# An early weight cast, a narrower wait and two earlier low parts in a Strassen-form attention and feed-forward kernel

## The chip, the cores and the metric

The kernel runs on one core of one Trainium2 chip. The metric is the device time of one execution in microseconds (us); lower is better. A number of executions are timed and the median is told; one more is recorded by the hardware profiler, and all rows shown here are of that one.

## What is computed

Attention with a soft cap, then two feed-forward layers, all in float32. The second and third steps take nearly all of the matrix work:

```python
scores = cap * np.tanh(scores / cap)            # 4 batches, 12 heads, 448 x 448
attn = exp(scores - max) / (sum + 1e-09)
x = (attn @ v)                                  # as 1792 tokens x 768
h = np.maximum(np.maximum(x @ w1, x @ w2), x @ w3)
x2 = h @ w_out                                  # 768 -> 768
g, val = x2 @ w_gate, x2 @ w_val                # 768 -> 1536
out = (g * sigmoid(g) * val) @ w_out2           # 1536 -> 768
```

## The kernel before

After the attention part, which the change does not touch, the work is 60 **quads**, two times 30 (one half of the tokens each). A quad is a 2 x 2 block product done with seven products in place of eight (Strassen in Winograd's form); product i of quad q is called (q, i) here, i from 0 to 6. Each product has three chunks of depth 128, and each chunk three matmuls of 448 columns, because a float32 operand is split into a high and a low part: `hi*hi`, `hi*lo`, `lo*hi`. So a product is 9 matmuls and a quad 63.

What a product needs:
- **A weight.** SyncE loads it into `whole` (a ring of 10), ScalarE casts the high part (`weights_hi`, L588), GpSimd subtracts to get the low part (L461). The load of weight n is issued once product n - 10 is done. ScalarE casts weight n + 8 at product n of its own list.
- **Operands.** A stage's input is seven blocks per chunk, in the order B11, T1, T2, T3, B22, B21, T4 (`SPLIT_ORDER`). T1 to T4 are differences that VectorE makes (L742 to L753). Each is split as well: ScalarE makes the high part (`operand_hi`, L606), VectorE the low part (`operand_lo`, L760: two inputs in SBUF).
- **A free PSUM bank.** Products 0 to 3 go to banks 0 to 3; products 4, 5 and 6 are added onto banks 0, 2 and 3, after ScalarE has copied bank 0 out (`take_p1`, L612), VectorE has made `u4` (L858) and VectorE has made the block C22 (L864). Ahead of these VectorE makes `u2` (L851) from product 1 and ScalarE's copy. So within a quad VectorE's chain is u2, u4, C22, later C12 (L880) and C21 (L887); `u2` and `u4` gate (q, 5), and C22 gates (q, 6).

Nothing reorders the work at run time: each engine runs the list that the code writes out, and semaphores join them. A quad whose result feeds the next stage is called a chunk's last quad; its event e is (stage, chunk). The seven low parts of event e are spread by hand over VectorE's list: some right after T4 is made, two after the next quad's `u2`, two after its `u4`, and what is left after its C22.

A **stage start** is a quad with q mod 30 in 0, 9, 12, 18, 27. The stage's last chunk of operands is not ready then, so TensorE runs the first two chunks of (q, 0) to (q, 3), then of (q+1, 0) and (q+1, 1), and then the third chunks. It so needs weight (q+1, 1) early.

Kinds of quads in one half: 0 to 8 "max" (three projections, their maximum), 9 to 11 "out1", 12 to 17 "gate" and "val" in turn, 18 to 20 "part", 21 to 26 gate and val again, 27 to 29 "out". In a gate quad ScalarE's list has the tanh of C22 (L644) ahead of the weight cast of product 5. In an out1 quad ScalarE copies C11 straight into the operand block B11 (`take_c11`, L628).

Of the kernel before, what the change touches and what calls it, by code (L numbers as in the profile page):

```python
# [28 lines left out]
PROD = 7  # L29
BANK_OF = (0, 1, 2, 3, 0, 2, 3)  # L30
J_B11, J_T2, J_T1, J_T3, J_B21, J_B22, J_T4 = range(PROD)
# [72 lines left out]
def event_of(q):  # L104

    s, k = divmod(q, QUADS)
    kind, g, n = kind_of(q)
    if kind == "max" and n == 2:
        return KCH * (STAGES * s + ST_H) + g
    if kind == "out1":  # L110
        return KCH * (STAGES * s + ST_X2) + g
    if kind == "val":
        return KCH * (STAGES * s + (ST_GV0, ST_GV1)[n]) + g
    if kind == "out" and s + 1 < SUPER:
        return KCH * STAGES * (s + 1) + g
    return None


def build(nc, w_in, qk_in, v_in, cap_in, out):
    ctx = ExitStack()  # L120
    with ctx:
# [452 lines left out]
        @block.scalar  # L574
        def _(act):
            def weigh(a):
                act.wait_ge(score_done, a + 1)
                if a >= NP:
                    act.wait_ge(value_done, a - NP + 1)
                nc.scalar.activation(prob[:, a % NP, :, :], score_banks(a)[0:KEYS, :, 0:SEQ], ACT.Tanh,  # L580
                                     scale=tanh_scale[0:KEYS, 0:1]).then_inc(tanh_done, 1)
                act.wait_ge(tanh_done, a + 1)
                nc.scalar.activation(prob[:, a % NP, :, :], prob[:, a % NP, :, :], ACT.Exp,  # L583
                                     scale=cap[0:KEYS, 0:1]).then_inc(exp_done, 1)

            def weights_hi(n):
                act.wait_ge(w_loaded[n % RING], 16 * (n // RING + 1))
                nc.scalar.activation(w_hi[:, n % RING, :], whole[:, n % RING, :],  # L588
                                     ACT.Copy).then_inc(w_hi_done, 1)

            def operand_hi(e, n):
                j = SPLIT_ORDER[n]
                if n == 0:
                    if operands_free(e) > 0:
                        act.wait_ge(prod_done, operands_free(e))
                    elif e // KCH == ST_H:
                        act.wait_ge(norm_done, ALL_PAIRS)
                        act.wait_ge(value_done, STEPS)
                        for i in range(2):
                            act.wait_ge(sum_stored[i], 16 * QUADS // 2)  # L600
                if j in (J_T1, J_T2, J_T3, J_T4):
                    act.wait_ge(t_done, 4 * (e - EARLY) + (J_T1, J_T2, J_T3, J_T4).index(j) + 1)
                else:
                    act.wait_ge(*block_ready(e, j))
                hi = operands(e // KCH)[0]
                nc.scalar.activation(hi[:, j, e % KCH, :], blk[:, j, :], ACT.Copy).then_inc(op_hi_done, 1)  # L606

            def take_p1(q):
                act.wait_ge(prod_done, PROD * q + 1)
                if q > 0:  # L610
                    act.wait_ge(u2_done, q)
                nc.scalar.activation(p1[:, :], bank(q, 0), ACT.Copy).then_inc(p1_taken, 1)  # L612

            def take_c11(q):
                s, k = divmod(q, QUADS)
                kind, g, n = kind_of(q)
                b = bank(q, 0)
                if kind == "max" and n == 0:
                    act.wait_ge(prod_done, PROD * q + 5)
                    if g > 0:  # L620
                        act.wait_ge(*c11_taken(q - 1))
                    elif s > 0:
                        act.wait_ge(out_stored[0], 16 * s * KCH)
                    nc.scalar.activation(sig[:, 0, :], b, ACT.Copy).then_inc(max_first, 1)
                elif kind == "out1":
                    act.wait_ge(prod_done, PROD * q + 5)
                    act.wait_ge(op_lo_done, PROD * (event_of(q) - EARLY))
                    nc.scalar.activation(blk[:, J_B11, :], b, ACT.Copy).then_inc(x2_first, 1)  # L628
                elif kind == "part":
                    act.wait_ge(prod_done, PROD * q + 5)  # L630
                    if g > 0:
                        act.wait_ge(part_stored[0], 16 * part_index(q))
                    else:
                        act.wait_ge(valued, 4 * gv_index(q - 1) + 2)
                    nc.scalar.activation(sig[:, 0, :], b, ACT.Copy).then_inc(part_first, 1)

            def gate_tanh_of(q, n):
                i = 4 * gv_index(q) + n
                if i >= 2:
                    act.wait_ge(gated, i - 1)  # L640
                source = (sig[:, 3, :], bank(q, 0), sig[:, 1, :], sig[:, 2, :])[n]
                act.wait_ge(*((c22_done, q + 1), (prod_done, PROD * q + 5), (c12_done, q + 1),
                              (c21_done, q + 1))[n])
                nc.scalar.activation(tmp[:, n % 2, :], source, ACT.Tanh, scale=0.5).then_inc(gate_tanh, 1)  # L644

            act.wait_ge(cap_loaded, 16)
            nc.scalar.activation(table_warm[:, :], cap[:, :], ACT.Tanh)
            act.wait_ge(scale_done, 2)
            for a in range(STEPS):
                weigh(a)  # L650
                n = 2 * (a // CH - RING_FROM - 1) + a % CH - 1
                if a % CH in (1, 2) and 0 <= n < FIRST_HI:
                    weights_hi(n)
            for n in range(PROD):
                operand_hi(EARLY, n)
            for q in range(ALL_QUADS):
                kind = kind_of(q)[0]
                e = event_of(q)
                loaded = kind == "out"
                for i in range(PROD):  # L660
                    if FIRST_HI <= PROD * q + i + AHEAD < PROD * ALL_QUADS:
                        weights_hi(PROD * q + i + AHEAD)
                    if i == 0:
                        take_p1(q)
                    if kind == "gate":
                        if i == 4:
                            gate_tanh_of(q, 0)
                            gate_tanh_of(q, 1)
                        elif i == 5:
                            gate_tanh_of(q, 2)  # L670
                        elif i == 6:
                            gate_tanh_of(q, 3)
                    elif i == 4:
                        take_c11(q)
                    if e is not None and not loaded:
                        if i == 4:
                            operand_hi(e, 0)
                        elif i == 5:
                            for n in range(1, 5):
                                operand_hi(e, n)  # L680
                        elif i == 6:
                            for n in range(5, PROD):
                                operand_hi(e, n)
                if e is not None and loaded:
                    for n in range(PROD):
                        operand_hi(e, n)

        @block.vector
        def _(dve):
# [220 lines left out]
            for q in range(ALL_QUADS):  # L910
# [17 lines left out]
                if e is None or kind == "out":  # L928
                    add_c12(q)
                    add_c21(q)  # L930
                    if kind == "gate":
                        gate_of(q, 2)
                        gate_of(q, 3)
                    if e is not None:
                        differences(e)
                        last_difference(e)
                        early = 4 if e % KCH == KCH - 1 else 2
                        for n in range(early):
                            operand_lo(e, n)
                        left = [(e, n) for n in range(early, PROD)]  # L940
                elif e % KCH == KCH - 1:
                    add_c12(q)
                    differences(e)
                    for n in range(4):
                        operand_lo(e, n)
                    add_c21(q)
                    last_difference(e)
                    left = [(e, n) for n in range(4, PROD)]
                else:
                    add_c12(q)  # L950
                    differences(e)
                    add_c21(q)
                    last_difference(e)
                    operand_lo(e, 0)
                    left = [(e, n) for n in range(1, PROD)]
    return nc


# [43 lines left out]
```

## Time and profile before

| what | value |
|---|---|
| median of 3 runs | 1079.63 us (1076.57 to 1082.3) |
| the profiled execution, its own time | 1078.85 us |
| its span, first to last instruction | 1077.1 us |
| TensorE matmuls, busy | 1015.7 us, 94% of the span |
| VectorE, GpSimd, ScalarE busy | 730.6, 616.4, 558.4 us |
| mean granted TensorE clock | 0.982 |

TensorE is the engine that works nearly all the time. Matmul records overlap (each is shown as 0.36 us while the next starts 0.20 us later), so busy time says little of how dense the stream is; what tells is the distance between starts, and the idle time that the trace gives ahead of an instruction with the engine that ended it.

### The profile page before, as it was taken

How to read it: one execution, taken by the hardware profiler on the slowest of the kernel's cores; microseconds unless marked ns; L12 is line 12 of the kernel's file. 1: busy time of each engine (PE TensorE's matmuls, PEld its weight loads, DVE VectorE, ACT ScalarE, POOL GpSimd, SP SyncE). 2: the span in 40 equal slices, each digit the busy share in tenths (PEclk: the TensorE clock that was granted, in tenths of full speed). 3: DMA queues.
4: the chain of work that ended last, by engine and by line, in shares of the span. 5: the costliest groups of instructions: out<-in, count | busy, mean ns of one | idle time of the engine just before them, and what ended most of it. 6: DMA issues, size and time to landing. Idle time of an engine off the chain costs nothing. (4 is left out here: it accounts for less than half of the span.)

```text
span 1077.1 us, 14096 instructions
## 1 busy us (share of the span) xinstructions
PE 1015.7 (94%) x4740; PEld 830.4 (77%) x4740; DVE 730.6 (68%) x956; ACT 558.4 (52%) x936; POOL 616.4 (57%) x562
## 2 busy tenths in 40 slices
PE   7999998796999988999999978999999999999998
PEld 4555554354999977998999967899987899899987
DVE  4788789495567467886348869565658688437864
ACT  6888885792344354544434543443435545444532
POOL 5455547476666554764656645564746666555643
PEclk9999999798999999999999999999999999999999
DMA  7989984944433332432643367333323333453336
GB/s 223 311 291 327 323 284 157 329 146 158 132 110 109 105 95 67 132 107 78 197 142 110 109 205 253 101 109 111 105 86 104 96 109 106 144 166 107 110 120 211
DMA packets 120791, 169.24 MB, mean 157 GB/s; under 512 B 10128, under 2 KB 117648, under 8 KB 120720
## 3 DMA queue, kind: packets, MB, share of 16 engines
q1 hardware_dynamic: 120720, 168.34, 49.8%
q8 instruction: 39, 0.64, 0.3%
q14 instruction: 32, 0.26, 0.1%
HBM read 130.94 MB, written 37.36 MB: 156 GB/s over the span
## 5 line engine op out<-in xcount | busy, mean ns | idle before, releaser
L461 POOL TENSOR_TENSOR w_lo<-whole,w_hi 128x384 fp32r<-128x384 f32 x420 | 473.8, 1145 | 333.2 <-ACT w_hi L588 332.1
L588 ACT ACTIVATE w_hi<-whole 128x384 fp32r<-128x384 f32 x420 | 215.1, 519 | 233.1 <-DMA whole<-s_store 139.0
L538 PE MATMUL acc<-a_hi,w_hi 128*128 128x448 f32 x882 | 325.3, 369 | 8.9 <-POOL w_lo L461 7.6
L538 PE MATMUL acc<-a_lo,w_hi 128*128 128x448 f32 x882 | 322.7, 366 | 0.0
L538 PE MATMUL acc<-a_hi,w_lo 128*128 128x448 f32 x882 | 322.6, 366 | 0.0
L538 PEld LDWEIGHTS acc<-a_hi,w_hi 128*128 128x128 f32 x882 | 166.1, 188 | 29.8 <-issue 8.3
L538 PEld LDWEIGHTS acc<-a_hi,w_lo 128*128 128x128 f32 x882 | 166.1, 188 | 13.2
L538 PEld LDWEIGHTS acc<-a_lo,w_hi 128*128 128x128 f32 x882 | 166.1, 188 | 12.8
L490 PE MATMUL acc<-prob,v_one 112*128 112x448 f32 x384 | 163.3, 570 | 5.8 <-DMA v_one<-v_in 5.8
L538 PE MATMUL acc<-b_hi,w_hi 128*128 128x448 f32 x378 | 142.8, 378 | 23.1 <-POOL w_lo L461 10.6
L538 PE MATMUL acc<-b_hi,w_lo 128*128 128x448 f32 x378 | 139.6, 369 | 0.0
L538 PE MATMUL acc<-b_lo,w_hi 128*128 128x448 f32 x378 | 139.5, 369 | 0.0
L490 PEld LDWEIGHTS acc<-prob,v_one 112*128 112x128 f32 x384 | 71.8, 197 | 79.1 <-issue 72.3
L760 DVE TENSOR_TENSOR b_lo<-blk,b_hi 128x448 fp32r<-128x448 f32 x126 | 117.5, 970 | 0.4
L606 ACT ACTIVATE b_hi<-blk 128x448 fp32r<-128x448 f32 x126 | 69.1, 575 | 82.5 <-DVE blk L742 41.9
L580 ACT ACTIVATE prob<-acc,tanh_scale 112x896 f32<-112x896 f32 x96 | 95.8, 997 | 30.7 <-PE acc L476 30.0
L851 DVE TENSOR_TENSOR u<-acc,p 128x448 f32<-128x448 f32 x60 | 37.5, 625 | 108.6 <-PE acc L538 91.2
L538 PEld LDWEIGHTS acc<-b_hi,w_hi 128*128 128x128 f32 x378 | 72.0, 191 | 39.3 <-issue 14.1
L583 ACT ACTIVATE prob<-prob,cap 112x896 f32<-112x896 f32 x96 | 100.1, 1042 | 3.2
L438 POOL TENSOR_TENSOR sum_w<-raw_w 128x384 f32<-128x384 f32 x30 | 32.3, 1075 | 97.1 <-DMA raw_w<-w_in 97.1
L538 PEld LDWEIGHTS acc<-b_hi,w_lo 128*128 128x128 f32 x378 | 72.0, 190 | 6.0
L538 PEld LDWEIGHTS acc<-b_lo,w_hi 128*128 128x128 f32 x378 | 72.2, 191 | 5.3
(61 smaller groups left out, 984.9 us busy)
## 6 DMA issues: line engine op xcount, KB each, us to landing
whole<-s_store SPq DMA_DIRECT2D x240, 192.0 KB, 2.3
whole<-w_in SPq DMA_DIRECT2D x180, 192.0 KB, 2.4
raw_w<-w_in SPq DMA_DIRECT2D x30, 768.0 KB, 8.1
s_store<-sum_w SPq DMA_DIRECT2D x30, 768.0 KB, 6.0
qk_raw<-qk_in SPq DMA_DIRECT2D x24, 448.0 KB, 5.2
v_one<-v_in SPq DMA_DIRECT2D x24, 224.0 KB, 3.8
part_store<-sig SPq DMA_DIRECT2D x24, 224.0 KB, 2.8
sig<-part_store SPq DMA_DIRECT2D x24, 224.0 KB, 3.8
```

Of the source, the lines that this page charges most:

```text
L438: nc.gpsimd.tensor_tensor(s1, a21, a22, ALU.add).then_inc(sum_done, 1)
L461: nc.gpsimd.tensor_tensor(w_lo[:, n % RING, :], whole[:, n % RING, :], w_hi[:, n % RING, :].bitcast(F32), ALU.subtract).then_inc(w_lo_done, 1)
L490: last = nc.tensor.matmul(value_banks(g)[:, h, 0:SEQ], v_one[:, g % 2, c, h * P:(h + 1) * P], prob[:, a % NP, h, :], start=(c == 0), stop= ...
L538: last = nc.tensor.matmul(bank(q, BANK_OF[i]), w[:, n % RING, cols], m[:, i, c, :], start=(i < 4 and c == 0 and t == 0), stop=(c == KCH - ...
L580: nc.scalar.activation(prob[:, a % NP, :, :], score_banks(a)[0:KEYS, :, 0:SEQ], ACT.Tanh, scale=tanh_scale[0:KEYS, 0:1]).then_inc(tanh_don ...
L583: nc.scalar.activation(prob[:, a % NP, :, :], prob[:, a % NP, :, :], ACT.Exp, scale=cap[0:KEYS, 0:1]).then_inc(exp_done, 1)
L588: nc.scalar.activation(w_hi[:, n % RING, :], whole[:, n % RING, :], ACT.Copy).then_inc(w_hi_done, 1)
L606: nc.scalar.activation(hi[:, j, e % KCH, :], blk[:, j, :], ACT.Copy).then_inc(op_hi_done, 1)
L760: nc.vector.tensor_tensor(lo[:, j, e % KCH, :], blk[:, j, :], hi[:, j, e % KCH, :].bitcast(F32), ALU.subtract).then_inc(op_lo_done, 1)
L851: nc.vector.tensor_tensor(u2[:, :], bank(q, 1), p1[:, :], ALU.add).then_inc(u2_done, 1)
```

## The change

Three edits, in the lists of ScalarE and VectorE. No instruction is added or taken away.

```diff
@@ take_c11, kind "out1"
-                    act.wait_ge(op_lo_done, PROD * (event_of(q) - EARLY))
+                    act.wait_ge(op_lo_done, ready(J_B11, event_of(q) - 1))
@@ ScalarE, the loop over quads
+            cast = FIRST_HI
             for q in range(ALL_QUADS):
...
                 for i in range(PROD):
-                    if FIRST_HI <= PROD * q + i + AHEAD < PROD * ALL_QUADS:
-                        weights_hi(PROD * q + i + AHEAD)
+                    ahead = AHEAD
+                    if i == PROD - 1 and (q + 1) % QUADS in STARTS:
+                        ahead = AHEAD + 1
+                    while cast <= PROD * q + i + ahead and cast < PROD * ALL_QUADS:
+                        weights_hi(cast)
+                        cast += 1
                     if i == 0:
                         take_p1(q)
@@ VectorE, end of a quad that makes a chunk other than a stage's last
                     differences(e)
                     add_c21(q)
                     last_difference(e)
-                    operand_lo(e, 0)
-                    left = [(e, n) for n in range(1, PROD)]
+                    for n in range(3):
+                        operand_lo(e, n)
+                    left = [(e, n) for n in range(3, PROD)]
```

ScalarE, from quad 8 into quad 9 (the first stage start after quad 0). `w_hi` is a weight's high part, `b_hi` an operand's, `p` the copy of bank 0. Before:

```order
L588 ACTIVATE w_hi<-whole 128x384 x4
L606 ACTIVATE b_hi<-blk 128x448
L588 ACTIVATE w_hi<-whole 128x384
L606 ACTIVATE b_hi<-blk 128x448 x4
L588 ACTIVATE w_hi<-whole 128x384
L606 ACTIVATE b_hi<-blk 128x448 x2
L588 ACTIVATE w_hi<-whole 128x384
L612 ACTIVATE p_54<-acc 128x448
```

and with the change:

```order
L588 ACTIVATE w_hi<-whole 128x384 x4
L606 ACTIVATE b_hi<-blk 128x448
L588 ACTIVATE w_hi<-whole 128x384
L606 ACTIVATE b_hi<-blk 128x448 x4
L588 ACTIVATE w_hi<-whole 128x384 x2
L606 ACTIVATE b_hi<-blk 128x448 x2
L612 ACTIVATE p_54<-acc 128x448
```

The cast of weight (10, 1) now stands ahead of the last two operand parts (B21 and T4), and no longer behind them.

VectorE, from the end of quad 2 (chunk 0 of the next stage is made) through quad 3, C22 of which is the row at L864. `u_55` is u2, `u_56` is u4, `b_lo` an operand's low part. Before:

```order
L887 TENSOR_TENSOR tmp<-acc,u_55 128x448
L771 TENSOR_TENSOR blk<-tmp,sig 128x448
L753 TENSOR_TENSOR blk<-blk 128x448
L760 TENSOR_TENSOR b_lo<-blk,b_hi 128x448
L851 TENSOR_TENSOR u_55<-acc,p_54 128x448
L760 TENSOR_TENSOR b_lo<-blk,b_hi 128x448 x2
L858 TENSOR_TENSOR u_56<-acc,u_55 128x448
L760 TENSOR_TENSOR b_lo<-blk,b_hi 128x448 x2
L864 TENSOR_TENSOR sig<-acc,u_56 128x448
L760 TENSOR_TENSOR b_lo<-blk,b_hi 128x448 x2
L880 TENSOR_TENSOR sig<-acc,u_55 128x448
```

and with the change (line numbers are five higher behind the edits on ScalarE):

```order
L892 TENSOR_TENSOR tmp<-acc,u_55 128x448
L776 TENSOR_TENSOR blk<-tmp,sig 128x448
L758 TENSOR_TENSOR blk<-blk 128x448
L765 TENSOR_TENSOR b_lo<-blk,b_hi 128x448 x3
L856 TENSOR_TENSOR u_55<-acc,p_54 128x448
L765 TENSOR_TENSOR b_lo<-blk,b_hi 128x448 x2
L863 TENSOR_TENSOR u_56<-acc,u_55 128x448
L765 TENSOR_TENSOR b_lo<-blk,b_hi 128x448 x2
L869 TENSOR_TENSOR sig<-acc,u_56 128x448
L885 TENSOR_TENSOR sig<-acc,u_55 128x448
```

Three low parts now stand ahead of u2 where one stood, and six of the seven after the first stand ahead of C22 where four stood. This holds after every chunk that is not a stage's last and not made by an out quad, so for quads 3, 6, 10, 11, 14, 16, 23 and 25 of each half (those that follow the chunk's quad). Of these 16 places 4 follow a max quad, 4 an out1 quad and 8 a val quad.

## Rows read from the trace of the kernel before

**Rows 1.** TensorE's waits for weights from 360 us on: total us, times, longest.

```profile
PE acc L538 <- POOL w_lo L461: 16.6, 11, 2.3
```

**Rows 2.** TensorE in order of time: start us, us, instruction [idle before, releaser].

```profile
383.88 0.44 PE L538 MATMUL acc<-b_hi,w_hi 128*128 128x448 f32 x1 [1.76 <-POOL w_lo L461]
...
425.77 0.44 PE L538 MATMUL acc<-a_hi,w_hi 128*128 128x448 f32 x1 [0.73 <-POOL w_lo L461]
...
428.35 0.44 PE L538 MATMUL acc<-a_hi,w_hi 128*128 128x448 f32 x1 [1.11 <-POOL w_lo L461]
...
677.40 0.71 PE L538 MATMUL acc<-a_hi,w_hi 128*128 128x448 f32 x1 [2.27 <-POOL w_lo L461]
```

**Rows 3.** ScalarE, then GpSimd, in order of time at the start of quad 9.

```profile
378.47 0.51 ACT L588 ACTIVATE w_hi<-whole 128x384 fp32r<-128x384 f32 x1
381.02 1.24 ACT L606 ACTIVATE b_hi<-blk 128x448 fp32r<-128x448 f32 x2 [2.04 <-DVE blk L771]
382.16 0.51 ACT L588 ACTIVATE w_hi<-whole 128x384 fp32r<-128x384 f32 x1
...
379.06 1.45 POOL L461 TENSOR_TENSOR w_lo<-whole,w_hi 128x384 fp32r<-128x384 f32 x1 [3.96 <-ACT w_hi L588]
382.75 0.99 POOL L461 TENSOR_TENSOR w_lo<-whole,w_hi 128x384 fp32r<-128x384 f32 x1 [2.24 <-ACT w_hi L588]
```

**Rows 4.** SyncE's issue of weight (10, 1), and loads of 370 to 380 us.

```profile
374.08 0.33 SPq L330 DMA_DIRECT2D whole<-s_store  x1
...
DMA to landing us min/median/max: 2.3/2.3/2.4
```

**Rows 5.** VectorE in order of time, four low parts, C21 and its maximum.

```profile
377.40 2.23 DVE L760 TENSOR_TENSOR b_lo<-blk,b_hi 128x448 fp32r<-128x448 f32 x4
...
380.19 0.79 DVE L771 TENSOR_TENSOR blk<-tmp,sig 128x448 f32<-128x448 f32 x1
```

**Rows 6.** VectorE in order of time, from the first low part to C22 of quad 3.

```profile
302.30 1.44 DVE L760 TENSOR_TENSOR b_lo<-blk,b_hi 128x448 fp32r<-128x448 f32 x1
303.93 0.62 DVE L851 TENSOR_TENSOR u<-acc,p 128x448 f32<-128x448 f32 x1 [0.18 <-ACT p L612]
304.47 1.99 DVE L760 TENSOR_TENSOR b_lo<-blk,b_hi 128x448 fp32r<-128x448 f32 x2
306.39 0.61 DVE L858 TENSOR_TENSOR u<-acc,u 128x448 f32<-128x448 f32 x1
306.92 2.26 DVE L760 TENSOR_TENSOR b_lo<-blk,b_hi 128x448 fp32r<-128x448 f32 x2
309.11 0.61 DVE L864 TENSOR_TENSOR sig<-acc,u 128x448 f32<-128x448 f32 x1
```

**Rows 7.** GpSimd in order of time, quad 3, then quad 14.

```profile
303.49 9.29 POOL L461 TENSOR_TENSOR w_lo<-whole,w_hi 128x384 fp32r<-128x384 f32 x7 [0.22 <-ACT w_hi L588]
...
452.98 6.57 POOL L461 TENSOR_TENSOR w_lo<-whole,w_hi 128x384 fp32r<-128x384 f32 x5 [0.22 <-ACT w_hi L588]
```

**Rows 8.** TensorE in order of time, around the start of product (3, 6).

```profile
309.29 0.37 PE L538 MATMUL acc<-a_lo,w_hi 128*128 128x448 f32 x1
309.50 0.36 PE L538 MATMUL acc<-a_hi,w_lo 128*128 128x448 f32 x1
309.77 0.47 PE L538 MATMUL acc<-a_hi,w_hi 128*128 128x448 f32 x1
```

**Rows 9.** ScalarE in order of time, quad 14: tanh of C22, then weight (15, 6).

```profile
459.31 0.58 ACT L644 ACTIVATE tmp<-sig 128x448 f32<-128x448 f32 x1 [2.63 <-DVE sig L864]
...
460.22 0.51 ACT L588 ACTIVATE w_hi<-whole 128x384 fp32r<-128x384 f32 x1
```

**Rows 10.** VectorE's u2 of quad 10 and TensorE at product (11, 6).

```profile
398.31 0.62 DVE L851 TENSOR_TENSOR u<-acc,p 128x448 f32<-128x448 f32 x1 [1.57 <-issue]
...
418.08 0.47 PE L538 MATMUL acc<-b_hi,w_hi 128*128 128x448 f32 x1 [0.75 <-DVE blk L864]
```

**Rows 11.** Stretch; us busy PE, PEld, DVE, ACT, POOL; PEclk, DMA share, GB/s.

```profile
677.40:680.81 3.41, 3.41 (x9) 3.06 (x10) 0.00 (x0) 0.00 (x0) 0.00 (x0) 0.51 0.02 5
```

## The prediction

> **What bounds the kernel now.** I read the page first: TensorE works 94% of the span, so what counts is where its stream of matmuls has holes. Two things are to be seen. A matmul starts about 0.20 us after the one before (309.29 to 309.50) although each is shown as 0.36 us long [rows 8], so an idle time of x in the trace is a loss of about x + 0.16. And the list of TensorE's waits from 360 us on has one large entry: 11 waits for a weight's low part from GpSimd, 16.6 us [rows 1]. In order of time all 11 stand at stage starts: six of 1.76 us (quads 9, 18, 27, 39, 48, 57; the first is shown), one of 2.27 (quad 30), and a pair of 0.73 and 1.11 at quads 12 and 42 [rows 2]. In all they cost 16.6 + 11 x 0.16 = 18.4 us.
>
> Why the weight is late shows on ScalarE at quad 9 [rows 3]. It is done with weight (10, 0) at 378.98, idles 2.04 us until VectorE delivers the maximum of C21, makes the parts of B21 and T4, and casts weight (10, 1) only at 382.16; GpSimd makes its low part from 382.75 to 383.74, and TensorE goes on at 383.88 [rows 2]. The weight was in memory long before: its load was issued at 374.08 and such loads landed in 2.3 us [rows 4].
>
> The second thing is a place without a hole. Product (3, 6) starts at 309.77, its predecessor at 309.50 [rows 8], so TensorE lost under 0.1 us there; but VectorE's C22, which releases it, ran from 309.11 to 309.72 [rows 6]. C22 comes at the last moment. The same pattern stands at all 12 places where such a quad follows a max or a val quad; 309.77 is the first. Whatever is put ahead of C22 there is paid in full by TensorE.
>
> **First edit: the weight cast ahead of B21 and T4.** Nothing is added, one cast of 0.51 us moves. In quad 8 it now fills part of ScalarE's 2.04 us of idling, at 378.98, so nothing behind it moves: B21's part waits for VectorE until 381.02 as before [rows 3], and the next copy of bank 0 waits for TensorE. The new wait that it can add is that for the load, which stands ready at 376.4 [rows 4]. It is in the list ahead of no DMA issue. GpSimd takes weight (10, 0) until 380.5 [rows 3]. VectorE's maximum, waiting since 380.19, took 0.79 us instead of 0.62 [rows 5], so it has its turn first, to 380.98; then GpSimd works 0.99 us, TensorE follows 0.14 us later as it did at 383.88, at 382.11. Without a hole it would have gone on at 383.88 - 1.92 = 381.96. So 0.15 us, rounded up to 0.2, stays at each of the six places. Quad 30 and the two pairs have more room (at 12 and 42 the second edit helps, below). Gain: 18.4 - 6 x 0.2 = **17.2 us**.
>
> **Second edit: C11 of an out1 quad waits for one low part.** At quad 10 C11's copy came late, since it waited for all low parts, and behind it in ScalarE's list stood the operand parts and a weight. TensorE itself does not wait for them there. It pays in the two following quads, together with the third edit.
>
> **Third edit: two low parts ahead of u2, so six in place of four ahead of C22.** What does a low part cost? The trace has two prices.
> - Bare, with GpSimd idle: four in 2.23 us, the last 0.62 long, so one each 0.54 us [rows 5].
> - With GpSimd at work: from u4 at 306.39 to C22 at 309.11, u4 and two low parts took 2.72 us [rows 6], so 1.36 a piece with u4 hidden. GpSimd worked without a pause then, seven low parts of weights in 9.29 us, 1.33 each, where one alone takes 0.99 [rows 7, 3]. The two engines take turns: 0.45 us for VectorE, 0.9 for GpSimd.
>
> I take the second, because GpSimd has a backlog over the whole stretch: its seven run from 303.49 to 312.78 in quad 3 [rows 7]. The first low part ended at 303.74 and u2 started at 303.93 [rows 6], so the room ahead of u2 is 0.2 us. With six low parts, three pairs of 2.72, C22 starts at 303.74 + 8.16 = 311.9, not 309.11: 2.8 us later. TensorE meets it in two steps, 1.9 us at (3, 5), since u4 now ends at 309.8 and that product began at 307.9 (309.77 less nine steps), and 0.9 at (3, 6). That holds for the 4 places behind a max quad: 11.2 us. Behind a val quad comes a gate quad, and there ScalarE casts weight (15, 6) only after the tanh of C22 [rows 9]; GpSimd's backlog is five pieces, not seven [rows 7], so the last of the six low parts is bare: 2.8 - 0.8 = 2.0 us, at 8 places: 16.0 us. Together **+27.2 us**. What the two low parts leave behind C22 is empty time for VectorE; TensorE cannot earn it back, since no wait of before hangs on these two low parts.
>
> The Trainium skill, "SBUF — State Buffer", section "Who interferes with whom", says that a VectorE instruction with two SBUF inputs and a GpSimd instruction that reads SBUF exclude one another for a whole instruction, and that one with a single SBUF input (u2 and u4 read PSUM and one SBUF tile) does not. By that rule the added low parts cost a GpSimd turn each, as in my sum; were the port shared without turns, the bare price would hold. The trace agrees with it, 1.36 against 0.54 us.
>
> At the four out1 places there is more room: VectorE idled 1.57 us ahead of u2 of quad 10 [rows 10], behind ScalarE's list. T1 waits for GpSimd's turn and T2 for another; two turns of 1.36 against 1.57 of room make u2 1.15 us later, and C22 of quad 10 some 1.4. In quad 11 C11 is not late any more, the differences come about 1 us earlier, and the wait for C22 at (11, 6), 0.75 + 0.16 + 0.1 us [rows 10], goes. Net +0.4 a pair of quads, **+0.8** for both; bounds -1.0 each if the two parts are bare, +1.4 if quad 11 gains nothing. That quads 12 and 42 get their weights in time rests on this: with two low parts fewer behind C22 and no wait of C11, the parts up to B22 are made about 2 us earlier (two parts of 0.6 and C11's copy and the rest of a turn), against holes of 0.73 and 1.11.
>
> **The clock.** After two of the holes at stage starts (quads 30 and 39) the granted clock was 0.51, the lower of the two levels, for about 3.4 us; nine matmuls took 3.41 us [rows 11] where nine steps of 0.204 are 1.84: 1.6 us lost each. Both holes go: -3.1. The new holes of 1.9 us are as long as the six of 1.76 were (1.92 from start to start), one of which had this behind it; 12 of them make two: +3.1. I enter **0**, bounds -3.1 and +16.
>
> **Sum**, against the profiled execution's own 1078.85 us: 1078.85 - 17.2 + 27.2 + 0.8 = 1089.7. That execution lay 0.8 us below the median of the runs shown, so I forecast a median of 1090 us, 1% slower.
>
> **The rivals.**
> - *Bare low parts (faster).* If VectorE gets its two added parts through without giving GpSimd turns, C22 comes 2 x 0.54 - 0.2 = 0.9 us later at 12 places, +10.6; the out1 quads gain 2.0, the clock 3.1: 1078.85 - 17.2 + 10.6 - 2.0 - 3.1 = 1067. For it: T1 of quad 3 did take 0.56 us, after u2. Against it: GpSimd had just finished then, and each second low part of a pair took the full turn [rows 6]. The change is faster when a place costs under (17.2 - 0.8) / 12 = 1.4 us. Chance 0.12.
> - *One turn, not two (no change).* T1 slips in behind B11's part ahead of GpSimd: 1.36 + 0.54 - 0.2 = 1.7 us a place, +20.4, clock about -1.5, 1080.5. Against it: GpSimd's piece was already waiting at 303.49 when B11's part ended at 303.74. Chance 0.13.
> - *The clock follows (slower still).* Half of the new double holes are followed by the low clock: 6 x 1.6 in place of 3.1, 1096. For it: at (q, 5) and (q, 6) a second hole follows after 1.8 us of work in 4 of 12. Chance 0.12.
> - *The first edit does not do what it says.* TensorE waits at the stage start for an operand or a load in place of the weight, and 17 us stay: 1107. Against it: the first low part of the last chunk is ready by 378.0 and needed after 383. Chance 0.03.
> - *As forecast*: 0.60, its own range 1084 to 1094 (0.2 us off at each of 12 places is 2.4, one clock stretch 1.6).
>
> **How the numbers follow.** About 0.5%, 5.4 us, is what a measurement of this kernel can tell from no change. Slower: 0.60 less a little, plus 0.12 and 0.03, 0.72. Same: 0.13 and a little, 0.14. Faster: 0.14. The range leaves out the bare case and the failed first edit and the upper end of the clock: 1076 to 1098.
>
> **What would show it.** In the profile after: weight waits on L538 down from 16.6 to about 1 us; TensorE's waits for u4 (L863) up by some 12 x 1.8 us and for C22 (L869) by about 4 x 0.8; low parts (L765) in quad 3 at a pitch of 1.36 ahead of u2; C22 of quad 3 about 8.2 us after its first low part's end. Wrong would be: u2 of quad 3 less than 1.5 us later than now against TensorE's product (3, 0); or an idle GpSimd beside the added parts.

## The result and the profile after

| | before | changed |
|---|---|---|
| median of 14 runs | 1078.6 us (1075.67 to 1082.3) | 1086.0 us (1083.3 to 1088.89) |
| ratio | 1 | 1.0071, 95% interval 1.0057 to 1.0084 |
| profiled execution, span | 1077.1 us | 1084.2 us |
| mean granted TensorE clock | 0.982 | 0.984 |

The change makes the kernel slower by 0.7%, 7.4 us by the medians. The forecast was 1090 us and slower, in a range of 1076 to 1098. One run of e6_memset_lows (below) took 1239.64 us at a granted clock of 0.753, far above its fellows, and is left out of that kernel's median and ratio.

The page of the changed kernel, its first part and two of its groups (line, engine, operation; busy us, mean ns of one; idle us before them and what ended it):

```profile
PE 1017.4 (94%) x4740; PEld 829.8 (77%) x4740; DVE 749.2 (69%) x956; ACT 559.3 (52%) x936; POOL 617.5 (57%) x562
...
L461 POOL TENSOR_TENSOR w_lo<-whole,w_hi 128x384 fp32r<-128x384 f32 x420 | 476.0, 1152 | 338.7 <-ACT w_hi L588 338.0
...
L765 DVE TENSOR_TENSOR b_lo<-blk,b_hi 128x448 fp32r<-128x448 f32 x126 | 127.1, 1053 | 0.0
```

The number of instructions is the same on every engine. VectorE is busy 18.6 us longer than before (749.2 against 730.6): not work, but mostly waiting inside its low parts. Those of `b_lo` had a mean of 970 ns before and are busy 9.6 us longer, those of `a_lo` (the other operand buffer) 6.7 us longer.

TensorE's waits from 360 us on in the changed kernel, the view of [rows 1]:

```profile
PE acc L538 <- DVE u L863: 23.0, 13, 2.4
PE acc L538 <- ACT p L612: 4.0, 1, 4.0
PE acc L538 <- DVE sig L869: 1.2, 2, 0.6
PE acc L538 <- DVE blk L869: 1.2, 2, 0.6
PE acc L538 <- DVE tmp L869: 0.6, 1, 0.6
```

The entry for weights (16.6 us, 11 waits) is gone altogether, and the one for u4, which was 4.2 us in 4 waits, is now 23.0 us in 13. One set of holes was traded for a larger one.

**Quad 3.** VectorE, GpSimd and TensorE in order of time, where before had [rows 6], [rows 7] and [rows 8]:

```profile
302.79 4.15 DVE L765 TENSOR_TENSOR b_lo<-blk,b_hi 128x448 fp32r<-128x448 f32 x3
306.86 0.61 DVE L856 TENSOR_TENSOR u<-acc,p 128x448 f32<-128x448 f32 x1
307.39 2.24 DVE L765 TENSOR_TENSOR b_lo<-blk,b_hi 128x448 fp32r<-128x448 f32 x2
309.56 0.61 DVE L863 TENSOR_TENSOR u<-acc,u 128x448 f32<-128x448 f32 x1
310.10 2.23 DVE L765 TENSOR_TENSOR b_lo<-blk,b_hi 128x448 fp32r<-128x448 f32 x2
312.25 0.61 DVE L869 TENSOR_TENSOR sig<-acc,u 128x448 f32<-128x448 f32 x1
...
303.97 9.21 POOL L461 TENSOR_TENSOR w_lo<-whole,w_hi 128x384 fp32r<-128x384 f32 x7 [0.23 <-ACT w_hi L588]
...
310.23 0.47 PE L538 MATMUL acc<-a_hi,w_hi 128*128 128x448 f32 x1 [1.70 <-DVE u L863]
...
312.92 0.47 PE L538 MATMUL acc<-a_hi,w_hi 128*128 128x448 f32 x1 [0.61 <-DVE sig L869]
```

The three low parts ahead of u2 start 1.36 us apart. From their start at 302.79 to C22 at 312.25 are 9.46 us; before, from 302.30 to 309.11, it was 6.81: 2.65 us later. Measured from the start of product (3, 0), which is at 298.76 before and at 299.25 in the changed kernel, C22 is 2.65 us later too. TensorE meets it in two steps, 1.9 us at (3, 5) and 0.9 at (3, 6).

**Quad 9's stage start.** ScalarE and GpSimd, where before had [rows 3]:

```profile
384.30 0.92 ACT L588 ACTIVATE w_hi<-whole 128x384 fp32r<-128x384 f32 x2
386.85 0.58 ACT L606 ACTIVATE b_hi<-blk 128x448 fp32r<-128x448 f32 x1 [1.62 <-DVE blk L776]
...
384.89 2.80 POOL L461 TENSOR_TENSOR w_lo<-whole,w_hi 128x384 fp32r<-128x384 f32 x2 [3.96 <-ACT w_hi L588]
```

Both casts stand in ScalarE's idle time, and GpSimd makes the two low parts without a pause.

**By quad.** TensorE's starts tell where each microsecond went. For each quad I took the time from the start of (q, 3) to that of (q+1, 3), less 0.2034 us for each matmul between: what is left is the time lost there. In us, for the quads where something is lost (28 and 29 are out quads, which no edit touches):

| quads | before | changed |
|---|---|---|
| 9, 18, 27, 39, 48, 57 | 2.54, 2.48, 2.52, 4.05, 2.46, 2.51 | 0.66, 0.61, 0.77, 0.64, 0.88, 0.61 |
| 12, 42 | 2.66, 2.67 | 0.32, 0.34 |
| 30 | 4.35 | 0.34 |
| 3, 6, 33, 36 (behind a max quad) | 0.13, 0.12, 0.11, 0.12 | 2.79, 2.80, 2.92, 2.60 |
| 14, 16, 23, 25, 44, 46, 53, 55 (behind a val quad) | 0.12, 0.11, 0.12, 0.10, 0.27, 0.09, 0.41, 0.10 | 1.97, 1.95, 1.96, 1.94, 4.12, 1.77, 2.23, 1.94 |
| 10, 40 | 2.28, 2.27 | 3.64, 3.48 |
| 11, 41 | 1.05, 1.04 | 0.20, 0.36 |
| 28, 29 | 7.28, 3.23 | 8.15, 1.15 |
| 0 | 3.24 | 4.24 |
| all of it, first to last matmul | 815.82 | 823.41 |

### The profile page after: what moved, and what is told of

It is laid out like the page before. It is cut to its first block and busy times, and to the rows that moved or that the text cites. A ratio compares the mean times of both kernels' runs of the same rounds, so it can differ in the third digit from the quotient of the medians.

```text
span 1084.2 us, 14092 instructions
## 1 busy us (share of the span) xinstructions
PE 1017.4 (94%) x4740; PEld 829.8 (77%) x4740; DVE 749.2 (69%) x956; ACT 559.3 (52%) x936; POOL 617.5 (57%) x562
## 5 line engine op out<-in xcount | busy, mean ns | idle before, releaser
L538 PE MATMUL acc<-b_hi,w_hi 128*128 128x448 f32 x378 | 141.9, 375 | 12.4 <-DVE u L863 5.9
L765 DVE TENSOR_TENSOR b_lo<-blk,b_hi 128x448 fp32r<-128x448 f32 x126 | 127.1, 1053 | 0.0
```

Of the source, the lines that this page charges most:

```text
L538: last = nc.tensor.matmul(bank(q, BANK_OF[i]), w[:, n % RING, cols], m[:, i, c, :], start=(i < 4 and c == 0 and t == 0), stop=(c == KCH - ...
L765: nc.vector.tensor_tensor(lo[:, j, e % KCH, :], blk[:, j, :], hi[:, j, e % KCH, :].bitcast(F32), ALU.subtract).then_inc(op_lo_done, 1)
```

## Experiments

### The first edit alone, the third alone, the first two

`e1_cast` has the loop with `cast` and `ahead` alone, `e2_lows` this alone:

```diff
-                    operand_lo(e, 0)
-                    left = [(e, n) for n in range(1, PROD)]
+                    for n in range(3):
+                        operand_lo(e, n)
+                    left = [(e, n) for n in range(3, PROD)]
```

and `e3_cast_wait` the first edit and the changed wait of `take_c11`.

> The first edit alone. My theory: the eleven waits for a weight's low part go and with them two stretches at the low clock, about 20 us in all, so 1078.6 - 20 = 1058 to 1060 us, and TensorE's list of waits has no entry, or under 2 us, for that low part. Rival (the edit gives little, another wait takes the place of the weight at the stage starts): 1070 us or more.

> The third edit alone. My theory: C22 comes 2.8 us later behind a max quad (4 places) and 2.0 later behind a val quad (8), 27 us, and the out1 quads lose 1.4 each at quads 10 and 40, so 1105 to 1109 us. Rival (bare low parts): the room of before swallows most of it, 1078 to 1090 us.

> The first and second edit without the third. My theory: 1056 to 1060 us, 2% faster than before; the second edit takes at most 1 us at each of quads 11 and 41 off the first edit alone. Rival (the edits need one another, the early low parts make the casts early): it stays above 1065 us.

| kernel | median | ratio to before, 95% |
|---|---|---|
| e1_cast | 1060.86 us | 0.9837, 0.9817 to 0.9857 |
| e2_lows | 1105.51 us | 1.0254, 1.0232 to 1.0276 |
| e3_cast_wait | 1060.0 us | 0.9827, 0.9806 to 0.9848 |

(before beside them: 1078.32 us.) The first edit takes 17.5 us off, the third alone adds 27.2. The rivals of both fall. The second edit beside the first alone changes nothing that can be told: quads 40 and 41 lose 2.28 and 1.05 us in e1_cast and 2.33 and 1.03 in e3_cast_wait, where up to 1 us less was expected at 41. TensorE's waits for u4 and for weights, in e1_cast and then in e2_lows:

```profile
PE acc L538 <- DVE u L863: 5.2, 4, 1.9
...
PE acc L538 <- POOL w_lo L461: 1.5, 2, 0.8
```

```profile
PE acc L538 <- DVE u L858: 24.4, 14, 2.4
PE acc L538 <- POOL w_lo L461: 13.2, 9, 1.8
```

One thing goes against the forecast. With the first edit alone two weight waits stay, and with the third alone nine of eleven. In e1_cast and e3_cast_wait quads 12 and 42 still lose 1.4 us each, and 0.3 in the changed kernel. In e3_cast_wait, which has the second edit, the entry is no smaller:

```profile
PE acc L538 <- POOL w_lo L461: 1.6, 3, 0.7
```

So it is not the second edit that lets those two quads have their weights in time, as the forecast said.

### The third edit with and without the second

`e12_no_wait_edit` is the changed kernel with the old wait of `take_c11`.

> First and third edit, the second left out. My theory as forecast: the second edit is what lets quad 11 and the stage starts at 12 and 42 recover, so this is 2 to 4 us slower than the changed kernel, 1088 to 1090 us. Rival (with the low parts done ahead of C22 the old wait is over by then anyway, so the second edit does nothing): 1086 us, within 1 us of the changed kernel.

Measured: 1088.44 us median, 1.0086 of before (1.0060 to 1.0112), 2.4 us over the changed kernel's 1086.0 by the medians, 1.6 by the ratios, whose intervals overlap: by time alone neither expectation is shown. The kernel has the first and third edits and lies 9.8 us over the before beside it (1078.64), as much as the two alone add up to, -17.5 + 27.2 = 9.7. By quad: 10 and 40 lose 4.19 and 3.62 (changed kernel 3.64 and 3.48), 11 and 41 lose 0.89 and 0.92 (0.20 and 0.36), and 12 and 42 lose 0.37 and 0.45. So where the third edit is in, the second is worth 1.3 us at quads 11 and 41. The 0.55 at quad 10 can't be put down to it, since a stretch at the low clock stands there in e12_no_wait_edit (407.40 to 410.70 us, granted clock 0.57) and none in the changed kernel. It has next to no part in 12 and 42. Those are cured by the third edit together with the first: with no low parts left behind C22 of quad 11, VectorE comes to C12 and the differences sooner. In e3_cast_wait C22, two low parts and C12 of quad 11:

```profile
414.90 0.62 DVE L869 TENSOR_TENSOR blk<-acc,u 128x448 f32<-128x448 f32 x1
415.56 2.00 DVE L765 TENSOR_TENSOR a_lo<-blk,a_hi 128x448 fp32r<-128x448 f32 x2
417.49 0.61 DVE L885 TENSOR_TENSOR blk<-acc,u 128x448 f32<-128x448 f32 x1
```

and in the changed kernel C22 and C12:

```profile
421.88 0.61 DVE L869 TENSOR_TENSOR blk<-acc,u 128x448 f32<-128x448 f32 x1
422.82 0.62 DVE L885 TENSOR_TENSOR blk<-acc,u 128x448 f32<-128x448 f32 x1 [0.33 <-PE acc L538]
```

Product (12, 0) starts at 417.53 in the one and at 424.47 in the other, so against TensorE C12 comes 1.6 us sooner, and with it the differences, the operand parts made from them and ScalarE's casts behind those, of weight (13, 0) first (from 421.11 and from 426.45 us).

### One low part in place of two

```diff
-                    operand_lo(e, 0)
-                    left = [(e, n) for n in range(1, PROD)]
+                    for n in range(2):
+                        operand_lo(e, n)
+                    left = [(e, n) for n in range(2, PROD)]
```

with the first two edits.

> First and second edit, and one low part ahead of u2 in place of the two of the change (two stand there, five in all ahead of C22). My theory, a full turn with GpSimd for each low part: C22 comes 1.36 + 1.36 - 1.3 = 1.4 us later than before at 12 places, so 17 us above the kernel with the first two edits alone, 1074 to 1077 us. Rival (the cost comes only when there are two, as the room of 0.2 us plus slack takes one): under 1064 us.

Measured: 1069.89 us median, 0.9928 of before (0.9907 to 0.9948); 9.9 us over e3_cast_wait, not 17, and below the 1074 to 1077 that I expected. VectorE in quad 3:

```profile
301.18 2.80 DVE L765 TENSOR_TENSOR b_lo<-blk,b_hi 128x448 fp32r<-128x448 f32 x2
303.91 0.61 DVE L856 TENSOR_TENSOR u<-acc,p 128x448 f32<-128x448 f32 x1
304.44 2.27 DVE L765 TENSOR_TENSOR b_lo<-blk,b_hi 128x448 fp32r<-128x448 f32 x2
306.63 0.61 DVE L863 TENSOR_TENSOR u<-acc,u 128x448 f32<-128x448 f32 x1
```

Again 1.36 us a low part. By quad the 12 places lose 1.16 to 1.48 us more than in e3_cast_wait, 15.7 in all, near the 17 that I expected. What I had not counted is what the low part gives: quads 11, 12, 41 and 42 lose 1.1 us less each, 4.4 in all, and 28 and 29, which vary from trace to trace, 3.1 less. So the rival (one is free) falls by the quads, although the total lies between the two numbers.

### Taking GpSimd's reads away

Does the price come from GpSimd? `e5_memset` is the kernel before with this, and `e6_memset_lows` has the third edit as well. The weights' low parts are left out of the result in both.

```diff
-                nc.gpsimd.tensor_tensor(w_lo[:, n % RING, :], whole[:, n % RING, :],
-                                        w_hi[:, n % RING, :].bitcast(F32),
-                                        ALU.subtract).then_inc(w_lo_done, 1)
+                nc.gpsimd.memset(w_lo[:, n % RING, :].bitcast(F32), 0.0).then_inc(w_lo_done, 1)
```

> The kernel before, with GpSimd's subtraction for each weight's low part replaced by writing zeros there (GpSimd reads nothing; the weights' low parts are left out of the result). It is the base for the next run. With bare low parts of operands and a quick write the holes at the stage starts shrink and those of quads 10, 11, 40 and 41 go: 1055 to 1068 us by both theories.

> The same with the third edit (weights' low parts zero, as in the run before). My theory, the two low parts cost a turn of GpSimd's reading instruction each: without such instructions six low parts and u2, u4 take 6 x 0.54 + 2 x 0.54 = 4.3 us of the 6.0 that quad 3 had, so the edit costs at most 2 us over that kernel. Rival (it is VectorE's own list, or the order of semaphores, that makes C22 late): 15 to 27 us over it.

Measured: 0.9718 of before (0.9680 to 0.9756, median 1046.74 us) and 0.9731 (0.9699 to 0.9763, median 1050.39 us of three runs). With GpSimd's reads the third edit cost 2.5% of the kernel, 27 us; without them 1.4 us by the ratios and 3.7 by the medians, either less than the intervals tell. At most 2 us was expected, and 15 to 27 by the rival, which falls. The base came out faster than I had expected, 1047 where the range was 1055 to 1068. All 126 low parts of `b_lo` in e6_memset_lows (min, median, max ns), and quad 3 on VectorE:

```profile
L758 DVE TENSOR_TENSOR b_lo<-blk,b_hi x126: 614/618/622, 300.3 to 1017.7; 128x448 fp32r<-128x448 f32 x126
...
300.31 1.69 DVE L758 TENSOR_TENSOR b_lo<-blk,b_hi 128x448 fp32r<-128x448 f32 x3
301.94 0.62 DVE L849 TENSOR_TENSOR u<-acc,p 128x448 f32<-128x448 f32 x1
302.48 1.15 DVE L758 TENSOR_TENSOR b_lo<-blk,b_hi 128x448 fp32r<-128x448 f32 x2
303.55 0.62 DVE L856 TENSOR_TENSOR u<-acc,u 128x448 f32<-128x448 f32 x1
304.08 1.15 DVE L758 TENSOR_TENSOR b_lo<-blk,b_hi 128x448 fp32r<-128x448 f32 x2
305.15 0.62 DVE L862 TENSOR_TENSOR sig<-acc,u 128x448 f32<-128x448 f32 x1
```

The same list takes 4.84 us to C22 where it took 9.46, and TensorE does not wait: the four places behind a max quad lose nothing in either kernel. GpSimd did overlap the low parts while it wrote zeros:

```profile
302.32 0.42 POOL L461 MEMSET w_lo<- 128x384 f32 x1 [0.42 <-ACT w_hi L586]
303.16 0.93 POOL L461 MEMSET w_lo<- 128x384 f32 x2 [0.43 <-ACT w_hi L586]
```

Neither was lengthened by the other: GpSimd's 420 writes took 417 to 423 ns each. GpSimd's work is also shorter here, 0.42 us, so the run takes away both its reads and its backlog; the overlap from 302.48 to 302.74 us is what says that it is the reading instruction that excludes VectorE.

### A version that beats both

In out1 quads u2 waits for ScalarE's copy of bank 0, which stands behind the last operand parts in its list. `e13_p1_one` puts that copy ahead of them in every quad that makes a chunk other than a stage's last, and keeps one extra low part at quads 11 and 41:

```diff
+            def p1_early(q):
+                e = event_of(q) if q >= 0 else None
+                return e is not None and e % KCH != KCH - 1 and kind_of(q)[0] in ('out1', 'max', 'val', 'out')
...
-                    if i == 0:
+                    if i == 0 and not p1_early(q - 1):
                         take_p1(q)
...
                         elif i == 6:
+                            if p1_early(q):
+                                take_p1(q + 1)
                             for n in range(5, PROD):
                                 operand_hi(e, n)
                 if e is not None and loaded:
+                    if p1_early(q):
+                        take_p1(q + 1)
```

> A version built from what the runs showed: first and second edit, the third only as one low part ahead of u2 of quads 11 and 41, and ScalarE copies bank 0 of the next quad ahead of the last operand parts (ahead of all of them in an out quad), where that quad is not a stage start. Theory: against 1060 us of the first two edits, the holes of quads 10, 11, 12 and of the other half go (2.2 + 1.0 + 1.1 us, twice), 12 places gain 0.1, quad 28 loses a wait of 4 us for that copy but keeps VectorE's lateness (gain 1 to 3): 1047 to 1052 us. Rival (ScalarE's early copy delays the operand parts and gives it back): 1058 us or more.

Measured: 1056.11 us median, 0.9787 of before (0.9763 to 0.9811), 4 us under e3_cast_wait where 8 to 13 were expected. Quads 10 and 40 lose 0.13 and 0.18 (2.19 and 2.33 in e3_cast_wait), as expected. But 11 and 41 lose 1.95 each, more than without any of this, and the 12 places lose nearly 0.3 more each. VectorE and GpSimd in quad 3:

```profile
303.33 0.61 DVE L864 TENSOR_TENSOR u<-acc,p 128x448 f32<-128x448 f32 x1
303.86 2.53 DVE L773 TENSOR_TENSOR b_lo<-blk,b_hi 128x448 fp32r<-128x448 f32 x2
...
303.53 7.79 POOL L461 TENSOR_TENSOR w_lo<-whole,w_hi 128x384 fp32r<-128x384 f32 x6 [0.62 <-ACT w_hi L588]
```

u2 no longer waits for ScalarE, but the copy, put forward in ScalarE's list, puts back the cast of a weight. From the start of product (3, 0), GpSimd's piece begins 0.40 us later than in e3_cast_wait (5.12 against 4.72 us) and the low part T1 0.25 us earlier (5.45 against 5.70). So T1 has to wait for that piece, and the pair takes 2.53 us where it took 1.99 [rows 6]: u4 comes 0.27 us later, not 0.2 sooner. The two runs that follow keep the early copy where it paid, behind out1 and out quads; `e15_p1_some_one` has the extra low part at 11 and 41, `e14_p1_some` has not.

> First and second edit, no low part moved, and the early copy of bank 0 behind out1 and out quads alone. Theory from the quads of the run before: 12 places get back 0.26 us each that the early copy cost there (VectorE's u2 came 0.2 earlier and fell into another turn of GpSimd), quads 11 and 41 lose their hole of 2.0 down to 0.6, quads 12 and 42 go back from 0.3 to 1.4 us: 1052 to 1055 us. Rival (the early copy was worth nothing and the 4 us of that run came from the one low part): 1058 us or more.

> The same with one more low part ahead of u2 of quads 11 and 41. Theory: 1.4 us more at quads 11 and 41, 1.1 less at 12 and 42, so within 1 us of the run without it, 1052 to 1055 us. Rival (a low part there is free, as VectorE idles): 1 to 3 us faster than the run without it.

Measured: e14_p1_some 1051.33 us, 0.9757 of before (0.9736 to 0.9778); e15_p1_some_one 1050.52 us, 0.9756 (0.9730 to 0.9782). Quads 11 and 41 lose 0.18 and none without the low part and 1.79 and 1.95 with it; 12 and 42 lose 1.42 and 1.80 without and 0.31 with it. By these quads the low part costs 1 us net, by the medians it gains 0.8: within 1 us either way, as expected, and not enough to tell the rival (1 to 3 us faster) from it. Both kernels came out just under the 1052 to 1055 expected, as quads 11 and 41 lost next to nothing without the low part where 0.6 was expected. Either is 2.4% faster than before and 3% faster than the changed kernel. What is most of the rest in e14_p1_some, in TensorE's waits:

```profile
PE acc L538 <- DVE u L871: 4.3, 1, 4.3
PE acc L538 <- POOL w_lo L461: 1.8, 2, 1.1
```

## Why the prediction was right, term by term

The measured column is the difference of the two by-quad columns above. By those the matmuls of the two profiled executions differ by 7.6 us; the forecast was +10.8 with the clock at zero.

| term of the sum | forecast | measured |
|---|---|---|
| stage starts (9 quads) | -17.2 | -18.0 |
| behind a max quad (4 places) | +11.2 | +10.6 |
| behind a val quad (8 places) | +16.0 | +15.0 |
| quads 10, 11, 40, 41 | +0.8 | +1.0 |
| clock | 0 (-3.1 + 3.1) | -1.5 |
| the rest | 0 | +0.5 |

The stage starts are the sum of -12.4 (six quads), -4.7 (12 and 42) and -4.0 (30), less the two stretches at the low clock at 1.55 each, which are in the clock's row. The val row is 16.6 less one stretch of 1.55 at quad 44. The clock's row has two stretches gone and that one come. The rest is small by luck: quad 0 loses 1.0 us more, quad 28 0.9 more and three other quads 0.8 together, and quad 29 loses 2.1 less, and the forecast had none of these. Quad 0's row holds a further stretch at the low clock, in quad 1 (265.80 to 269.10 us, granted clock 0.55), which the kernel before did not have.

- **Where the kernel waits, and why.** Right: all weight waits went, as ScalarE's and GpSimd's rows at quad 9 show. I had left 0.2 us at six of them for VectorE's turn; from 360 us on TensorE waited for no weight at all.
- **C22 without slack, and a full turn a low part.** Right in mechanism and size: 1.36 us a low part in the changed kernel and in e8_one_low, 0.54 in e6_memset_lows. The mechanism is shown by taking GpSimd's reads away. The price was some 5% too high per place: 2.65 us measured at a max quad for 2.8, and 1.8 for 2.0 at seven of the val places, 2.3 at quad 44. In quad 3 C22 starts 8.03 us after the shown end of the first low part (304.22 us), where three pairs of 2.72 made 8.16: the next low part starts 0.07 us before that end, and the three pairs take 8.10. "The same pattern stands at all 12 places" was a little too strong: at quads 44 and 53 TensorE already lost 0.27 and 0.41 us before. The reason for the difference between the two kinds (GpSimd has five pieces, not seven, until the tanh of C22) shows in VectorE's last pair of quad 14, where the second low part is bare:

```profile
460.70 0.61 DVE L863 TENSOR_TENSOR u<-acc,u 128x448 f32<-128x448 f32 x1
461.23 1.41 DVE L765 TENSOR_TENSOR b_lo<-blk,b_hi 128x448 fp32r<-128x448 f32 x2
462.57 0.61 DVE L869 TENSOR_TENSOR sig<-acc,u 128x448 f32<-128x448 f32 x1
```

- **The second edit.** "That quads 12 and 42 get their weights in time rests on this" was wrong in its cause. The run without the second edit has them in time, and the one with the first two edits has not: it is the third edit that empties VectorE's list behind C22. The time was right, since both edits are in the change. "TensorE cannot earn it back" holds at the 12 places it was said of, and not behind an out1 quad: at quads 11, 12, 41 and 42 a moved low part earns 1.1 us each in e8_one_low.
- **The clock.** The size was off: I expected two new stretches at the low clock at the 12 places, and one came. It is behind the hole at (44, 5); a stretch of 3.50 us holds eleven matmuls, and the ten steps from 876.23 to 879.81 us take 3.58 us, 1.55 more than ten of 0.2034:

```profile
876.30:879.80 3.50, 3.50 (x11) 3.09 (x10) 2.52 (x5) 1.54 (x4) 1.01 (x1) 0.51 0.12 33
```

The clock is 1.5 of the 3.2 us by which the sum was too high. Of the 12 holes at (q, 5) it followed the longest, of 2.22 us; the other eleven, 1.44 to 1.97 us, had none behind them, nor had the two of 2.4 us at (10, 5) and (40, 5). In e2_lows and e12_no_wait_edit, which have the third edit too, it was again (44, 5) alone of the 12, but (10, 5) had the low clock behind it as well. So counting holes by their length, as my sum did, gave two stretches for one, and when the low clock comes is left open here.
- **The rivals.** Bare low parts: fallen (e2_lows, +27.2 us alone). One turn for two: fallen, two and three in a row took a turn each. The first edit without effect: fallen, -17.5 us alone. The clock following half of the new holes: not seen, one of 12.
- **The signs.** Weight waits went to none for the "about 1 us" forecast, low parts stood 1.36 us apart, and the waits for u4 rose by 22.2 us from 257 us on (4.2 to 26.4) for 21.6. The waits for C22 rose by 0.5 us (3.7 to 4.2) and not by 3.2: each of the four max places has its new wait, of 0.6 us, but those of 0.75 at (11, 6) and (41, 6) went.

## What to carry to other kernels

Before moving an instruction ahead of a sum or a copy that frees a buffer, look how far that release is from the moment when the waiting engine needs it: here C22 came within 0.1 us of need at ten places and late already at two, and everything put before it was paid in full. Price the moved instruction at what it takes in that place, beside what runs there, and not by its shortest time. And try the parts of a change apart: here one part was worth 17.5 us and another cost 27.2, so that the whole looked like a small loss.

## What the runs showed of the hardware

- VectorE's subtraction of two SBUF tiles (128 x 448) and GpSimd's (128 x 384) take strict turns when both have work waiting: one each in 1.36 us, three and six times in a row. From 300 us on in the traces of before, the changed kernel, e2_lows, e8_one_low and e13_p1_one neither engine was ever served twice while the other had waited 0.1 us or more. VectorE's sums with one input in PSUM (0.61 us) pass unhindered. A GpSimd instruction that only writes (0.42 us) takes no turn and delays none, as e6_memset_lows shows.
- Who goes first can hang on a hundredth of a microsecond. In quad 29, which no edit touches, GpSimd's first piece and VectorE's u2 and first low part start at the same distances in both kernels (0.44 and 0.98 us after GpSimd's), yet the pair takes 2.81 us in one and 1.97 in the other. VectorE and GpSimd in the kernel before, then in the changed one:

```profile
660.83 2.81 DVE L760 TENSOR_TENSOR a_lo<-blk,a_hi 128x448 fp32r<-128x448 f32 x2
...
659.85 4.66 POOL L461 TENSOR_TENSOR w_lo<-whole,w_hi 128x384 fp32r<-128x384 f32 x4 [6.29 <-ACT w_hi L588]
```

```profile
666.35 1.97 DVE L765 TENSOR_TENSOR a_lo<-blk,a_hi 128x448 fp32r<-128x448 f32 x2
...
665.37 5.17 POOL L461 TENSOR_TENSOR w_lo<-whole,w_hi 128x384 fp32r<-128x384 f32 x4 [6.42 <-ACT w_hi L588]
```

The low part comes just as GpSimd's first piece ends: GpSimd's second piece is shown from 660.82 and VectorE's low part from 660.83 us in the first, both from 666.35 in the second. One time the low part waits and the other time it gets in. TensorE loses 3.23 us in that quad in the first and 1.15 in the second, but only 0.84 of that is the turn; u2 also starts 7.44 us after product (29, 0) in the first and 6.23 in the second.
